# The forget gate of a scan moved from GpSimd to ScalarE

## The reference

```
sig = 1 / (1 + exp(-f_logit))
f = lower_bound + (1 - lower_bound) * sig
i = 1 - f
for t in range(S):            # h starts at 0 in each of the 4 sequences
    h = f[:, t] * h + i[:, t] * x[:, t]
    y[:, t] = h
```

## Time and profile before

| | |
|---|---|
| median of 3 runs | 2418.66 us (2417.88 to 2419.19) |
| the profiled execution | 2422.26 us, of which the span is 2420.5 us |
| scan stage (last operation of GpSimd's `score`) | up to about 190 us |
| VectorE busy over the first 190.5 us | 163.09 us |
| ScalarE, GpSimd busy over the first 190.5 us | 87.45 us, 110.24 us |
| DMA share over the first 190.5 us | 0.83 |

### The profile page before, as it was taken

How to read it: one execution, slowest core, us unless ns; L and a number is a source line. 1 busy time by engine, 2 the same in 40 slices (tenths; PEclk the granted TensorE clock), 3 DMA queues, 4 the chain that set the end, 5 groups by cost and what they waited for, 6 DMA issues and landing times. The chain is left out here.

```text
span 2420.5 us, 51866 instructions
## 1 busy us (share of the span) xinstructions
PE 2268.7 (94%) x18040; PEld 2114.1 (87%) x18041; DVE 1383.2 (57%) x3375; ACT 810.4 (33%) x2027; POOL 952.2 (39%) x1036
## 2 busy tenths in 40 slices
PE   7883699999999999999999869999999999999997
PEld 7882588888888888888898769999999999999997
DVE  8887876776767677686644433333343333333332
ACT  4440324242332424233333223333333333333332
POOL 5550233333333333333433353535353535335333
PEclk9995699999999999999999979999999999999999
DMA  7894111121211112121221131122121212111111
GB/s 275 289 315 150 53 43 64 42 69 40 71 41 45 66 40 68 42 71 38 77 79 42 43 101 47 42 78 77 43 76 45 78 44 73 47 44 42 41 46 37
DMA packets 86191, 182.95 MB, mean 76 GB/s; under 512 B 14318, under 2 KB 50929, under 8 KB 86066
## 3 DMA queue, kind: packets, MB, share of 16 engines
q0 software_dynamic: 31872, 85.58, 11.4%
q1 hardware_dynamic: 40722, 82.34, 9.7%
q10 hardware_dynamic: 13472, 13.37, 2.0%
HBM read 118.94 MB, written 64.13 MB: 76 GB/s over the span
## 5 line engine op out<-in xcount | busy, mean ns | idle before, releaser
L1853 DVE SCALAR_TENSOR_TENSOR m_hl<-m_hP,m_hh 128x256 fp32r<-128x256 f32 x664 | 274.9, 424 | 531.5 <-ACT m_hh L1812 460.3
L1812 ACT ACTIVATE m_hh<-m_hP 128x256 fp32r<-128x256 f32 x664 | 247.3, 384 | 514.8 <-PE m_hP L1763 510.8
L1085 ACT ACTIVATE m_hh<-m_hP 128x512 fp32r<-128x512 f32 (+1 forms) x320 | 189.8, 593 | 628.2 <-PE m_hP L956 617.0
L824 POOL DMA_INDIRECT y_rows<-spare,m_dest x164 | 182.0, 1110 | 537.4 <-DVE m_dest L1424 488.9
L1384 DVE SCALAR_TENSOR_TENSOR m_hl<-m_hP,m_hh 128x512 fp32r<-128x512 f32 (+1 forms) x320 | 218.5, 683 | 272.0 <-ACT m_hh L1085 253.4
L814 POOL DMA_INDIRECT spare<-h_rows,m_idx x164 | 192.0, 1171 | 56.9 <-issue 37.5
L1701 POOL DMA_INDIRECT m_xg<-y_rows,m_idx x170 | 167.9, 988 | 101.4 <-POOL m_idx L1697 69.5
L1712 POOL DMA_INDIRECT out_dram<-m_rows,m_dest x166 | 168.0, 1012 | 50.6 <-issue 50.6
L1697 POOL COPY m_idx<-rows_i 128x2 int32 (+1 forms) x85 | 15.6, 183 | 409.9 <-ACT m_meta L1816 389.2
L1774 PE MATMUL m_yP<-w_1h,m_hh 128*128 128x256 f32 x672 | 140.7, 291 | 1.3 <-DVE m_hl L1853 1.2
L1774 PE MATMUL m_yP<-w_0h,m_hh 128*128 128x256 f32 x656 | 137.4, 291 | 0.0
(11 more groups left out here) (297 smaller groups left out, 5693.4 us busy)
## 6 DMA issues: line engine op xcount, KB each, us to landing
spare<-in_moe_w_dram SPq DMA_DIRECT2D x32, 1024.0 KB, 6.1
f_in<-in_f_logit_dram SPq DMA_DIRECT2D x39, 512.0 KB, 4.5
x_in<-in_x_dram SPq DMA_DIRECT2D x39, 512.0 KB, 5.3
h_rows<-rows ACTq DMA_DIRECT2D x25, 512.0 KB, 4.5
h_rows<-spare SPq DMA_DIRECT2D x14, 512.0 KB, 6.2
m_xg<-y_rows,m_idx POOLq DMA_INDIRECT x170
out_dram<-m_rows,m_dest POOLq DMA_INDIRECT x166
spare<-h_rows,m_idx POOLq DMA_INDIRECT x164
```

The source lines that it names most:

```text
L824: pool.indirect_dma_start(dst[:, :], bass.IndirectOffsetOnAxis(ap=dest[:, k:k + 1].bitcast(U32), axis=0), rows[(i - 1) % 2][:, k, 0:ROW].b ...
L1085: act.activation(hh[f % 2][:, tokens(i)], hP[f % 2][:, tokens(i)], ACT.Relu).then_inc(hh_ready, 1)
L1812: act.activation(hh[f % AHEAD][:], hP[f % AHEAD], ACT.Relu).then_inc(hh_ready, 1)
L1853: dve.scalar_tensor_tensor(out=hl[f % AHEAD][:], in0=hP[f % AHEAD], scalar=0.0, in1=hh[f % AHEAD][:].bitcast(F32), op0=ALU.max, op1=ALU.su ...
```

## The change

ScalarE computes the gate right behind each sigmoid, as an activation with the function Identity, scale `lbc` and bias `lb`. It waits for its own sigmoid, and for the scan of the chunk two before. GpSimd's list keeps only the score additions. The store, which stands behind `gates` in ScalarE's list, keeps its place, and so do all the other waits: VectorE's `nix` still waits for `fg_ready`.

```diff
@@ ScalarE, gates(ch, b, nt), for each half d
                     act.activation(in_order(sig[:, d, 0:nt * P], nt), fP[d][:, 0:nt, :].rearrange("p k q -> p q k"),
                                    ACT.Sigmoid).then_inc(sig_ready, 1)
+                    if isinstance(ch, int) and ch == 0 and d == 0:
+                        act.wait_ge(small_in, 32)
+                        act.wait_ge(lbc_ready, 1)
+                    act.wait_ge(sig_ready, DH * ch + d + 1)
+                    if not first(ch):
+                        act.wait_ge(h_ready, DH * (ch - 2) + d + 1)
+                    act.activation(fg[:, b, d, 0:nt * P], sig[:, d, 0:nt * P], ACT.Identity,
+                                   bias=lb[:, d:d + 1], scale=lbc[:, d:d + 1]).then_inc(fg_ready, 1)
@@ GpSimd
             pool.tensor_scalar(lbc[:], lb[:], -1.0, 1.0, ALU.mult, ALU.add).then_inc(lbc_ready, 1)
-            pool.wait_ge(lbc_ready, 1)
-
-            def gates(ch, b, nt):
-                for d in range(DH):
-                    pool.wait_ge(sig_ready, DH * ch + d + 1)
-                    if not first(ch):
-                        pool.wait_ge(h_ready, DH * (ch - 2) + d + 1)
-                    alone(pool, passed)
-                    pool.tensor_scalar(fg[:, b, d, 0:nt * P], sig[:, d, 0:nt * P], lbc[:, d:d + 1], lb[:, d:d + 1],
-                                       ALU.mult, ALU.add).then_inc(fg_ready, 1)
...
-            gates(0, 0, TPC)
-            gates(1, 1, TPC)
             score(0, 0, TPC)
             with pool.Fori(1, full // 2) as k:
-                gates(2 * k, 0, TPC)
                 score(2 * k - 1, 1, TPC)
-                gates(2 * k + 1, 1, TPC)
                 score(2 * k, 0, TPC)
-            gates(full - 1, 0, TPC)
             score(full - 2, 1, TPC)
-            gates(full, 1, last_tiles)
             score(full - 1, 0, TPC)
             score(full, 1, last_tiles)
```

## The result

The changed kernel takes 2421.34 us (median of 22 runs, 2417.46 to 2428.35) against 2416.7 us before (22 runs beside them, 2414.78 to 2419.19). The ratio is 1.0023, with a 95% interval of 1.0017 to 1.0029. It is slower by 0.23%, some 4.6 us, where 6.9 us faster was forecast, and it lies outside the range of 2406 to 2420. Its runs also spread over 11 us, those of before over 4.4.

What follows compares the result with a forecast made beforehand. Bound: the gate ahead of VectorE in a two-chunk loop, no engine full. A pair falls from 8.95 to 8.46 us, 6.9 us over 14 pairs; 2418.66 - 6.9 = 2411.8 us, range 2406 to 2420.

Steps and rivals of the forecast that it cites:

- the one on the store: Scan stage: store issued behind both gates, 2.96 us after `halves`; up to 3.6 us loss in chunks 30 to 39, taken as nothing.
- One of the prediction's own signs of being wrong: Scan stage: the forecast is wrong if ScalarE's `halves` wait for stores more than once or twice.
- the sum: Scan stage, chunks 2 to 29: the new loop's steps added up to 8.46 us a pair, the middle of 8.39 and 8.53.
- GpSimd's gates and the scans: Scan stage: 80 tensor_scalars leave GpSimd, scans pair up in 2.67 us; VectorE's floor falls from 8.34 to 7.94 a pair.
- The gate, 0.79 us: ScalarE, scan stage: each moved gate takes 612 ns plus 180 for two column operands, bounds 0.61 and 0.97 us.
- The own wait, 0.05 us: ScalarE, scan stage: each gate starts 0.05 us after its own sigmoid ends; bounds 0.03 and 0.30 us.
- The named slower rival: ScalarE's wait for its own sigmoid is a real drain, 0.47 us a wait; chance 0.09, tables 0.02 of it.
- The chain of a pair, 8.39 to 8.53 us: Scan stage: loop from scan's end through `halves`, sigmoids, gates and VectorE back to scan's end, against 8.95 us before.
- No table load between sigmoid and Identity: ScalarE, scan stage: Identity is in every table set, so switching costs nothing; otherwise 205 us.
- VectorE idle between the two `nix`: Scan stage, first part: the second gate comes late, leaving VectorE idle some 0.26 us between the two `nix`.
- Chunks 30 to 39 stay at 4.6 us for want of data: Second part of the scan stage: DMA share 0.99, so no gain; 3.2 us more if that share hid room.
- 6.9 us in all: Scan stage, chunks 2 to 29: 0.49 us gained a pair over 14 pairs; nothing gained elsewhere.

Runs made afterwards that it cites:

- e1: The changed kernel with the store issued between the first sigmoid and the first gate, not behind both gates: 2412.8 us, ratio 0.9981.
- e6: e3 with the store behind the first sigmoid (four row buffers, ScalarE's list written out): 2412.6 us, ratio 0.9984.
- e3: The changed kernel with four row buffers in place of two and ScalarE's list written out, store still late: 2417.09 us, ratio 1.0006.
- e8: The changed kernel with ScalarE's list written out, no loop, two row buffers, same order and late store: 2418.11 us, ratio 1.0012.
- e2: The changed kernel with ScalarE's order sigmoid, sigmoid, store, gate, gate: 2408.37 us, ratio 0.9963.
- e7: Four row buffers, list written out, ScalarE's order as in e2: 2405.13 us, ratio 0.9949.
- e5: e4 with the store issued behind the first sigmoid: 2418.5 us, ratio 1.0004.
- e4: The kernel before, GpSimd's gates kept, plus two idle gate operations a chunk on ScalarE that nobody reads: 2424.49 us, ratio 1.0034.
- e10: Four row buffers, list written out, store issued between the two copies of the next chunk: 2421.69 us against 2422.98 before, ratio 0.9999.
- e9: e6 with each chunk's store behind the first sigmoid one chunk later: 2420.38 us against 2422.98 before, ratio 0.9988.

## Why the prediction was wrong

The step that failed is the one on the store: "I take nothing for the stretch, between these ends, since engines that are always busy lose no work when one transfer goes behind another", and, for the first part, "2.96 + 4.5 = 7.5, inside 8.46". The time of issue was about right (3.3 us after `halves` where 2.96 was forecast). The landing was not: the 4.5 us were measured for a store that leaves ahead of the loads (80.71 against 81.04), and were used for one that leaves behind them. There it is 5.4 us in the median and up to 10.0 in the first part (issued at 76.28, `halves` released at 86.26) and 11.2 in the second. And the premise of busy engines failed with the first late landing: ScalarE's list is in order, so loads stop too, and the DMA share sank to 0.73. The sign of the whole forecast hung on this step. One of the prediction's own signs of being wrong is met: `halves` waited for stores 12 times, where "once or twice" was the limit.

The result lies 11.5 us from the gain of 6.9 that was forecast. The store's place is worth 8.7 of it (e1 against the changed kernel). What is left, a gain of 4.1 in e1 in place of 6.9, lies in the chain itself: an undisturbed pair of e1 takes 8.77 us where the sum had 8.46, which is up to 4.3 us over 14 pairs.

Point by point, by the prediction's own steps:

- *GpSimd's gates and the scans.* Right. The scans of 512 columns average 1282 ns, 1359 before, and pair up in 2.67 us.
- *The gate, 0.79 us.* Right: 0.814, by the group of 78.

```profile
L345 ACT ACTIVATE fg<-sig,lb,lbc 128x512 f32<-128x512 f32 x78 | 63.5, 814 | 5.6
```

- *The own wait, 0.05 us.* Right without ScalarE's `Fori` (80.88 + 0.61 to 81.53 is 0.04 us in e6); with it 0.12 in one half of the pair (87.27 + 0.62 to 88.01), 0.03 in the other. The named slower rival, a wait of 0.47 us, did not happen; the slower outcome came from a step that had been priced at up to 3.6 us and held harmless by itself.
- *The chain of a pair, 8.39 to 8.53 us.* 8.40 in e3, e6 and e8, where ScalarE's list is written out; 8.70 in the changed kernel and 8.77 in e1, with `Fori`. The mechanism was right, 0.30 us that come with `Fori` are missing from the sum.
- *No table load between sigmoid and Identity.* Right. The scan stage has the two loads that it had, at 0.82 and 2.63 us, both ahead of the first sigmoid. So the trace agrees with what the Trainium skill, "ScalarE: Activation LUTs", Table sets, says of identity.
- *VectorE idle between the two `nix`.* Right in kind: 0.72 us in one half of the changed kernel's pair, 0.35 in each chunk of e6, where 0.26 was forecast. e2 removes it.
- *Chunks 30 to 39 stay at 4.6 us for want of data.* The reason does not hold, and whether the time stays depends on the variant. In e6 `nix` of the chunks stored one by one starts at 147.37, 151.54 and so on to 173.74: 26.37 us for 6 chunks, 4.40 each, against 4.63 before (154.24 to 182.05). e7 has 4.38. e1, with two buffers and the loop, stays at 4.64. The stretches from chunk 32 on, before and then e6, have the same DMA share and not the same GB/s:

```profile
154.24:170.20 15.96, 14.38 (x117) 13.14 (x116) 13.79 (x15) 7.52 (x15) 9.35 (x11) 1.00 1.00 345
...
147.37:165.02 17.65, 15.08 (x128) 14.22 (x127) 15.06 (x17) 14.90 (x25) 4.36 (x4) 1.00 1.00 357
```

  Of the 8.1 us by which e6's profiled execution, its fastest, reaches the routing sooner (185.14 against 193.23), 6.2 are gained by chunk 30 (138.97 against 145.19) and 1.9 behind it. A share of 0.99 was no proof of full engines. The estimate from the page "DMA: Bandwidth & Descriptors", Specifications, of the Trainium skill was 4.39 us a chunk and 2 us in all; by e6 it was nearer than the share.
- *6.9 us in all.* With the store early the move of the gates is worth 4.1 us in the loop (e1), and 4.0 with the list written out and four buffers (e6), though the undisturbed pair of e6 would give 7.7: not every pair is undisturbed. Putting the store late costs 8.7 us in the loop (e1 against the changed kernel), 5.7 with idle gates (e5 against e4), and 4.2 with four buffers (e6 against e3).

What stays open is why a single store takes 10 us or more. Part of it can be read. The store issued at 76.28 moved 427 of its 528 packets from 79 to 81 us. From 81 to 83, from 83 to 85 and from 85 to 87 us the stores' queue had these:

```profile
q10 hardware_dynamic: 15, 0.02, 2.2%
...
q10 hardware_dynamic: 11, 0.01, 1.6%
...
q10 hardware_dynamic: 7, 0.01, 0.9%
```

That is 33 packets, and a sixteenth of 528 is 33. From 84.0 to 85.4 us the DMA share was 0.07, about one sixteenth, while the store and the load issued at 79.18, which landed 6.9 us later, were both under way:

```profile
84.00:85.40 1.40, 0.45 (x5) 0.21 (x2) 0.00 (x0) 0.00 (x0) 0.00 (x0) 1.00 0.07 26
```

So the numbers fit one of the 16 DMA engines that still had its part of both transfers to do, while the other fifteen stood still. The records do not name the engine, and why it fell behind is not shown. The landing of 11.2 us is not of this kind alone: from 165 to 167 us, around it, the stores' queue had 22.8% and the loads' 31.4%, more than one engine could have.

## What to carry to other kernels

When an operation moves into an engine's list, count the DMA issues that stand behind it there, and ask of each who waits for its landing. A landing time read from a trace belongs to the moment at which that transfer is issued relative to the others; it can't be carried to another moment. Here the place of one store was worth 8.7 us, and the whole change with the store in a good place 4.1. A busy share near 1 is no proof that transfers can't go faster: at a share of 1.00 they moved 345 GB/s in one kernel and 357 in another.

## What the runs showed of the hardware

- A store of 512 KB lands in 3.5 us when it is issued 1.1 us ahead of two loads of 512 KB, and in 7.2 us when it is issued right behind them (medians, e6 and e3), with the loads slower too: `x_in` lands in 5.4 and 6.2 us. Its first packet moves 0.9 us after the issue in e6 and 4.0 us after it in e3, when the packets of the loads ahead of it have moved.
- The last sixteenth of a store can lag behind the rest: 33 of 528 packets came after 81 us, the last at about 85.8, in a store whose other packets had moved by then (changed kernel). The copy that waited for its landing stood still for 5.59 us.
- ScalarE's list in a `Fori` loop took 0.30 us more for a pair than the same list written out: 8.70 and 8.40 us (changed kernel and e8). What in the loop costs it is not shown.
- The third stage, whose code is the same in all kernels, is not equally long in each execution. From the first to the last product into `m_hP` with `w_1h` it took 850.3 to 852.5 us in nine profiled executions, 856.5 in e10, 856.6 before and 858.8 in e9. This is most of why the changed kernel's profiled span is only 6.1 us longer than before with a scan stage 11.4 us longer. So differences of 6 us between two profiled spans say nothing of the scan stage; its own end has to be read.
